# Key features times values: one tile shared by two heads, as two 64-row products on the halves of the array

## The reference, cut to what matters

```python
def phi(x):                                     # per head, x is 576 x 64
    proj = np.einsum('bhsd,df->bhsf', x, w_phi) # 576 x 128
    proj = proj - np.max(np.abs(proj), axis=-1, keepdims=True)
    return np.concatenate([np.exp(proj), np.exp(-proj)], axis=-1)
q_p, k_p = (phi(q), phi(k))
kv = np.einsum('bhsf,bhsd->bhfd', k_p, v)       # the product that is changed
z = np.sum(k_p, axis=2)
num = np.einsum('bhsf,bhfd->bhsd', q_p, kv)
den = np.einsum('bhsf,bhf->bhs', q_p, z)[..., None] + 1e-06
return (num / den)
```

## Time and profile before

| | us |
|---|---|
| median of 3 runs | 2069.24 |
| lowest, highest | 2067.35, 2069.4 |
| the profiled execution | 2066.68 |
| its span in the trace | 2064.9 |
| TensorE busy in it | 2032.0 (98%) |

### The profile page before, as it was taken

One profiled execution on the slowest core, in us unless ns is written; L12 is line 12 of the kernel. 1 busy time (PEld: TensorE's weight loads), 2 busy tenths in 40 slices (PEclk: granted clock), 3 DMA queues, 4 the chain that ended last, 5 costly groups with the idle time before them and its releaser, 6 DMA issues.

```text
span 2064.9 us, 31691 instructions
## 1 busy us (share of the span) xinstructions
PE 2032.0 (98%) x12658; PEld 1205.9 (58%) x12658; DVE 1008.8 (49%) x1606; ACT 696.3 (34%) x1372; POOL 174.3 (8%) x179
## 2 busy tenths in 40 slices
PE   7999999999999999999999999999999999899998
PEld 6888755555555555555555555555555565566775
DVE  6888855544444444444444444444444433644433
ACT  6666532232233332232233333322333332222221
POOL 0753300000000000000000000000000000211110
PEclk9999999999999999999999999999999999999999
DMA  7322111221122112212211221221122240731600
GB/s 215 70 62 66 43 61 63 82 82 41 41 82 82 42 56 102 87 41 82 83 41 42 82 82 43 96 104 45 41 82 82 82 184 21 275 144 45 272 26 8
DMA packets 93247, 169.38 MB, mean 82 GB/s; under 512 B 60454, under 2 KB 60582, under 8 KB 89776
## 3 DMA queue, kind: packets, MB, share of 16 engines
q1 hardware_dynamic: 89104, 157.92, 21.8%
q0 software_dynamic: 4000, 9.45, 1.4%
HBM read 126.19 MB, written 44.83 MB: 83 GB/s over the span
## 4 chain that ended last, share of the span: by engine, by line
PE 96%; DVE 1%; DMA 1%; SPq 1%; issue 0%; ACT 0%; POOL 0%; POOLq 0%; DVEq 0%
PE ps L653 36%; PE ps L672 36%; PE ps L854 6%; PE ps L838 4%; PE ps L602 3%; PE ps L615 3%; PE ps L840 2%; PE ps L581 2%; PE ps L590 1%; DMA arena<-in_k_dram 1%; PE ps L568 1%; PE ps L717 1%; PE ps L809 1%; PE ps L687 0%; SPq L352 0%
## 5 line engine op out<-in xcount | busy, mean ns | idle before, releaser
L653 PE MATMUL ps<-arena 128*128 128x384 f16 x4608 | 774.4, 326 | 0.7 <-issue 0.7
L672 PE MATMUL ps<-arena 128*128 128x512 f16 x3456 | 771.2, 380 | 0.0
L653 PEld LDWEIGHTS ps<-arena 128*128 128x128 f16 x4608 | 450.5, 98 | 312.6 <-issue 1.1
L672 PEld LDWEIGHTS ps<-arena 128*128 128x128 f16 x3456 | 338.5, 98 | 392.4 <-issue 2.2
L958 ACT ACTIVATE arena<-ps 128x384 f32<-128x384 f32 x384 | 188.5, 491 | 1019.8 <-PE ps L653 1015.8
L1253 DVE TENSOR_TENSOR arena<-arena 128x384 f16<-128x384 f32 x384 | 214.1, 558 | 313.0 <-ACT arena L962 312.1
L1308 DVE SCALAR_TENSOR_TENSOR arena<-ps,wt,arena 128x512 f32<-128x512 f32 x126 | 94.6, 751 | 436.8 <-PE ps L672 436.5
L962 ACT ACTIVATE arena<-ps 128x384 f16<-128x384 f32 x384 | 186.0, 484 | 0.0
L1133 DVE TENSOR_REDUCE wg<-arena 128x1 f32<-128x1024 f32 x128 | 154.8, 1211 | 28.5 <-DMA arena<-in_moe_w_dram 28.4
L1149 DVE SCALAR_TENSOR_TENSOR arena<-arena,wsc 128x1024 f16<-128x1024 f32 x124 | 158.5, 1278 | 0.8 <-ACT arena L924 0.6
L924 ACT ACTIVATE arena<-arena,wsc 128x1024 f16<-128x1024 f32 x124 | 142.6, 1150 | 1.9 <-DVE wsc L1080 1.9
(11 more groups left out here) (203 smaller groups left out, 1182.5 us busy)
## 6 DMA issues: line engine op xcount, KB each, us to landing
arena<-in_moe_w_dram SPq DMA_DIRECT2D x32, 2048.0 KB, 8.5
split_weights<-arena SPq DMA_DIRECT2D x16, 2048.0 KB, 7.4
arena<-split_weights SPq DMA_DIRECT2D x8, 4096.0 KB
arena<-in_q_dram SPq DMA_DIRECT2D x16, 288.0 KB, 3.5
arena<-in_k_dram SPq DMA_DIRECT2D x16, 288.0 KB, 3.9
arena<-in_v_dram SPq DMA_DIRECT2D x2, 2304.0 KB, 12.1
x_rows<-arena SPq DMA_DIRECT2D x18, 256.0 KB, 2.5
arena<-in_v_dram SPq DMA_DIRECT2D x32, 128.0 KB, 2.3
```

What stands on the lines that cost most here:

```text
L653: last = pe.matmul(o, ring[:, slot, sw, FF * c + 128 * j:FF * c + 128 * j + 128], xT[:, sx, c, BLK * blk:BLK * blk + BLK], start=(n == 0), ...
L672: last = pe.matmul(ps[:, Y_PS + tt, :], hbuf[:, blk % 2, sh, f, 128 * tt:128 * tt + 128], ring[:, slot, 2 + sw, D * f:D * f + D], start=(n ...
```

## The change

The shared tile is no longer multiplied twice with 128 rows (64 of them zeros in `vone`), but as two products with 64 rows each: partitions 0 to 63 for head 0, partitions 64 to 127 for head 1, one right after the other. The loop over the sign is now outermost: for each sign the four full tiles of head 0, the two halves, then the four full tiles of head 1. Head 1's sums move to bank 7, so the accumulator is banks 4 and 7 with 256 columns in each, and VectorE's copy reads these two pieces. The number of instructions stays: 20 products for a pair, of which 4 now have 64 rows. Loads, the zeros in `vone`, the waits and the signals stay.

```diff
-        KV_PS = ps[:, 4, :]
+        KV_PS = ps[:, 4:8:3, 0:256]
@@ keys_values
-                for x in range(2):
-                    for s in range(2):
-                        for n in range(MID + 1):
-                            last = pe.matmul(KV_PS[:, 128 * (2 * x + s):128 * (2 * x + s) + 128], kp[:, par, s, MID * x + n, :],
-                                             vone[:, par, (MID + 1) * x + n, :], start=(n == 0), stop=(n == MID))
+                def part(x, s, n, rows):
+                    return pe.matmul(KV_PS[:, x, 128 * s:128 * s + 128], kp[rows, par, s, MID * x + n, :],
+                                     vone[rows, par, (MID + 1) * x + n, :], start=(n == 0), stop=(n == MID))
+
+                every = slice(0, 128)
+                for s in range(2):
+                    for n in range(MID):
+                        part(0, s, n, every)
+                    part(0, s, MID, slice(0, 64))
+                    part(1, s, 0, slice(64, 128))
+                    for n in range(1, MID + 1):
+                        last = part(1, s, n, every)
                 last.then_inc(kv_done, 1)
@@ stationary
-                dve.tensor_copy(kvst.rearrange("p x s c -> p (x s c)"), KV_PS).then_inc(kvst_ready, 1)
+                dve.tensor_copy(kvst.rearrange("p x s c -> p x (s c)"), KV_PS).then_inc(kvst_ready, 1)
```

## The result

The changed kernel takes 2072.25 us (median of 20 runs, 2069.58 to 2074.21) against 2067.43 us for the kernel before in the same measurement (20 runs, 2065.33 to 2071.61). The ratio is 1.0025, with a 95% interval of 1.0019 to 1.0031: 0.25% slower, 4.8 us. The interval as a whole lies above 1, so the change does cost time; its lower end is just under the prediction's bound of 0.2%.

What follows compares the result with a forecast made beforehand. TensorE, busy for 98% of the span, was taken to bound the kernel. Each sign loses 0.39 us at switches and saves 0.22, so 14 pairs at 0.34 us add 4.8: 2069.2 to 2074.0 us, range 2068.5 to 2077.5.

Steps and rivals of the forecast that it cites:

- the prediction's bound of 0.2%: About 0.2% (4.1 us) is what a measurement of this kernel can tell from no change; slower by more: 0.67.
- The sum: Keys' product on TensorE: 0.34 us more for each of 14 pairs of heads, 4.8 us in all.
- The slots saved: Shared tile: a pair of half products needs two slots of 0.1118 us, not four, saving 0.22 us a sign.
- The rival in which the halves run in series: Half products don't run beside each other: no slots saved, all losses kept, +11 us, 2080.2; chance 0.07.
- steps 1 and 2: Into the halves: 0.20 us to the first half start (0.09 lost), then 0.21 to the second (0.10 lost).
- steps 3 and 4: Out of the halves: 0.21 us for one slot (0.10 lost), then a full product with open weight load (0.10 lost).
- Step 4: First full product behind the halves loads weights in the open: 377 ns against 275, 0.10 us lost; a transpose gives 0.06.
- the prediction's own test: The prediction is wrong if weight loads behind the half-row dip start ahead of their matmuls.
- The rival with one switch only: Full weights load ahead on the way out while halves run: -0.8 us, 2068.4, no change; chance 0.10.
- The pairs that pay: 14 of 16 pairs pay 0.34 us; the first two are covered by TensorE waits of 1.38 and 1.08 us.
- The edits at nothing: VectorE's copy from two banks, the order of heads and signs, and bank 7 were taken to cost zero.
- The free switch: Two slots saved for each sign and nothing lost at the switches: -6.3 us, 2062.9, 0.30% faster; chance 0.05.

Runs made afterwards that it cites:

- the changed kernel's second profile: The changed kernel profiled once more with no edit, to check the start-up before the third pair: 2071.78 us, against 2068.21 for the kernel before.
- the kernel with the halves apart: Changed kernel with one full product between the two half products of each sign, four separate half-row stretches a pair: 2087.58 us, ratio 1.0098 to the kernel before.
- the layout alone: Changed kernel's banks, order and split copy, but the shared tile again as two full 128-row products for each sign: 2067.68 us, ratio 0.9999 to the kernel before.
- one stay of four: Changed kernel with both signs' four half products side by side between eight and eight full products: 2065.83 us, ratio 0.9993 to the kernel before.
- beside the projection: Changed kernel with all sixteen full products first, then the four half products directly ahead of the projection: 2061.98 us, ratio 0.9975 to the kernel before.

## Why the prediction was right

**The sum.** +4.8 us were forecast and 4.8 us measured (interval 3.9 to 6.4). The forecast of 2074.0 us stood on a median of three runs, 2069.24; the median of 20 is 2067.43, which accounts for the 1.8 us between the forecast and 2072.25. The difference was right, the base was high by the scatter of three runs.

**The slots saved.** Two for each sign, as told: four half records in two starts, 137.67 and 137.88. The rival in which the halves run in series (14.15 us a pair) falls.

**The switch in and the first halves (steps 1 and 2).** 0.20 and 0.21 us expected, 0.21 and 0.21 in the records; the first half records last 0.38 us, 0.373 expected.

**The switch out and the open load behind it (steps 3 and 4).** 0.21 and 0.21 expected and found. Step 4 had two candidate rows, and the one of the same line and shape was right: the record has 0.38 us, and its load starts with it and not ahead, which was the prediction's own test. The rival with one switch only (13.3 us a pair) falls on this.

**The pairs that pay.** From the third pair's product to the last one it is 177.16 us against 172.75, that is 13 times 0.34, and the last product itself has 0.34 more; together 4.8. (The prediction has these pairs without a gap. From the third to the fourth it is 13.69 us in place of 13.37, with a short wait in it; in the changed kernel it is 14.03, so that pair pays its 0.34 too.) That the first two pairs pay nothing is shown best by the changed kernel's second profile: its second product is 0.34 us longer, TensorE's wait for ScalarE behind it is 0.72 us in place of 1.08, and the third pair starts 19.00 us behind the transposes, as in the kernel before. Before those transposes TensorE waits for a DMA that starts at 18.8 to 20.2 us, ahead of the first pair's product, in all four profiles of the two kernels; so the first pair's product can be longer by as much as that wait. Where both products are 1.54 us longer, in the kernel with the halves apart, the wait for the DMA is gone. Its total, 20.2 us for 14 x 1.54 = 21.6 expected, would have been 24.6 with all 16, outside its interval.

**Where there was luck.** The medians agree with the forecast to better than 0.1 us, while the interval runs from 3.9 to 6.4 us. Single executions move by more than that tenth: the lower clock alone is worth 2 us, and from the first expert product on the run takes 1828.5 to 1829.2 us in five of the eight profiles and 1826.8 to 1827.1 in three. The cause of the latter is open. The rhythm of 13.71 us and the records carry the account; the agreement of the medians to a tenth is chance.

**The edits at nothing.** The copy has 691 ns against 688; the layout alone gives a ratio of 0.9999 (0.9991 to 1.0008). Both as taken.

**The free switch**, the rival on the other side, falls with the stays of 0.385 us and comes true only where no switch is added. There the same edit of the products turns from 0.25% slower to 0.25% faster.

The five kernels fit one price: 0.39 us for going into the halves and back out, less 0.112 us for each slot that is saved. The fourth column is worked out from that price, the last is measured; the kernel before has 13.37.

| halves | stays added for a pair | slots saved | lost - saved, us | a pair measured, us |
|---|---|---|---|---|
| none (layout alone) | 0 | 0 | 0 | 13.38 |
| two stays of two (the change) | 2 | 4 | +0.33 | 13.71 |
| four stays of one | 4 | 0 | +1.56 | 14.91 |
| one stay of four | 1 | 4 | -0.06 | 13.32 |
| beside the projection | 0 | 4 | -0.45 | 12.93 |

How the 0.39 us divide into an array that empties and a weight load in the open is read off the records (0.09 to 0.10 and 0.10 each way), whose ends are modelled; no run separated the two. That the array empties is therefore an inference from the starts.

## What to carry to other kernels

Count how often a sequence goes between full-row and half-row work, not only how many slots the half rows save: here one stay cost 0.39 us, which is 3.5 fp32 slots of 0.112 us, so it needed four saved slots to pay. Put small half-row pieces beside a stage that is in the halves already, if the accumulators allow that order. And when a kernel already makes the switch somewhere, its start to start distances on a saturated engine can price the new one; here they did so to a few hundredths of a microsecond.

## What was not expected of the hardware

One thing: in the three forms that were run, the price of a stay doesn't depend on what runs in it. One product on one half (0.385 us a stay), two on both, and four on both (0.40 us between two stays and one) cost the same. The Trainium skill, TensorEngine Tiling (Array Packing), Key Properties, has the drain at a change of mode; these runs agree, with 0.20 to 0.21 us between starts across a change against 0.11 inside a mode. They add that weights aren't loaded ahead across it (a load at 138.09 for a matmul at 138.09), while inside the halves they are loaded ahead even from one stage to the next (150.11 for a matmul at 150.22).
